# Local and downsampled attention ahead of two MLP layers: values loaded for two batches at once, and the turning of the probabilities moved one unit later

## The reference

```python
q_d = q.reshape(B, H, Sd, factor, D).mean(axis=3)        # factor 4: 144 positions; k_d, v_d alike
out_up = np.repeat(sm_attn(q_d, k_d, v_d), factor, axis=2)
mask = np.abs(pos[:, None] - pos[None, :]) < factor      # a band of 7 keys around each query
out_local = softmax(where(mask, scale * q @ k.T, -1e9)) @ v
x = rows_of(out_up + out_local)                          # 2304 x 512
xn = x / rms(x) * rms_g
x = (silu(xn @ w_gate) * (xn @ w_val)) @ w_out           # 512 -> 1536 -> 512
y = square(relu(x @ w_in)) @ w_out2                      # 512 -> 2048 -> 512
```

## Time and profile before

| | |
|---|---|
| median of 3 runs | 962.38 us (960.26 to 963.59) |
| the profiled execution | 963.09 us, of which the span in the profile is 961.3 us |
| mean granted TensorE clock | 0.978 of full speed |
| PE busy | 926.8 us, 96% of the span |
| attention units, up to the first product | about 143 us of the span |

### The profile page before, as it was taken

One profiled execution on the slowest core, in us unless ns is written; L12 is line 12 of the kernel. 1 busy time (PEld: TensorE's weight loads), 2 busy tenths in 40 slices (PEclk: granted clock), 3 DMA queues, 4 the chain that ended last, 5 costly groups with the idle time before them and its releaser, 6 DMA issues.

```text
span 961.3 us, 17765 instructions
## 1 busy us (share of the span) xinstructions
PE 926.8 (96%) x6056; PEld 837.6 (87%) x6056; DVE 648.3 (67%) x960; ACT 447.9 (47%) x1149; POOL 588.7 (61%) x627
## 2 busy tenths in 40 slices
PE   5879989999999999999999999999999999999998
PEld 5657768999999999999999998989898998989896
DVE  5859995678986668876455776667875456745353
ACT  3758785644455634455444464424342324333221
POOL 2458677778778867877766775555654445453520
PEclk9979878999999999999999999999999999999999
DMA  6566211321211111111111122121112101030101
GB/s 178 180 206 210 82 35 33 89 77 54 68 45 44 45 45 45 45 45 45 44 46 54 54 69 88 44 88 45 45 36 97 45 23 44 23 110 23 45 1 65
DMA packets 57961, 63.94 MB, mean 67 GB/s; under 512 B 5904, under 2 KB 50832, under 8 KB 57488
## 3 DMA queue, kind: packets, MB, share of 16 engines
q1 hardware_dynamic: 56288, 61.63, 20.8%
q10 hardware_dynamic: 1584, 1.18, 0.4%
HBM read 58.07 MB, written 4.72 MB: 65 GB/s over the span
## 4 chain that ended last, share of the span: by engine, by line
PE 77%; DVE 3%; issue 1%; ACT 1%; POOL 0%; DMA 0%; ACTq 0%; DVEq 0%
PE bank L1437 42%; PE bank L1492 20%; PE bank L1467 14%; DVE xs L1079 1%; ACT wst L698 0%; ACT xs L739 0%; DVE vt L1146 0%; DVE prod L1152 0%; PE bank L1447 0%; DVE wst L1086 0%; POOL wst L576 0%; DMA out_dram<-xT 0%; DVE gt L1146 0%; DVE wo L1191 0%; ACT xT L822 0%
## 5 line engine op out<-in xcount | busy, mean ns | idle before, releaser
L1437 PE MATMUL bank<-xs,wst 128*128 128x384 f32 x2520 | 505.1, 340 | 4.1 <-DVE vt L1146 2.4
L1437 PEld LDWEIGHTS bank<-xs,wst 128*128 128x128 f32 x2520 | 442.7, 189 | 28.6 <-issue 8.5
L576 POOL TENSOR_TENSOR wst<-wraw,wst 128x256 fp32r<-128x256 f32 x240 | 223.9, 952 | 143.0 <-ACT wst L698 141.7
L1492 PE MATMUL bank<-wo,gs 128*128 128x512 f32 x864 | 218.4, 393 | 1.4 <-ACT xT L822 0.8
L1467 PE MATMUL bank<-hb,wo 128*128 128x512 f32 x864 | 189.1, 336 | 1.3 <-DVE hb L1164 1.3
L1492 PEld LDWEIGHTS bank<-wo,gs 128*128 128x128 f32 x864 | 160.4, 188 | 29.8 <-DVE gs L1185 1.1
L1467 PEld LDWEIGHTS bank<-hb,wo 128*128 128x128 f32 x864 | 146.0, 188 | 9.9 <-issue 1.6
L1146 DVE TENSOR_TENSOR vt<-u,bank 128x384 f32<-128x384 f32 x120 | 66.2, 552 | 126.1 <-PE bank L1437 125.8
L698 ACT CAST wst<-wraw 128x256 fp32r<-128x256 f32 x360 | 123.1, 407 | 1.9 <-DMA wraw<-w_dram 1.2
L559 POOL TENSOR_TENSOR wraw<-wraw,stage 128x256 f32<-128x256 f32 x60 | 48.9, 815 | 96.5 <-DMA wraw<-w_dram 96.5
L785 ACT ACTIVATE sig<-gt 128x384 f32<-128x384 f32 x72 | 37.9, 526 | 124.8 <-DVE gt L1146 123.7
(11 more groups left out here) (110 smaller groups left out, 1054.5 us busy)
## 6 DMA issues: line engine op xcount, KB each, us to landing
wraw<-w_dram SPq DMA_DIRECT2D x180, 128.0 KB, 2.3
stage<-w_dram SPq DMA_DIRECT2D x60, 128.0 KB, 2.1
woraw<-w_dram SPq DMA_DIRECT2D x28, 256.0 KB, 3.0
vquad<-v_dram SPq DMA_DIRECT2D x16, 288.0 KB
out_dram<-xT SPq DMA_DIRECT2D x18, 256.0 KB, 2.9
vwin<-v_dram SPq DMA_DIRECT2D x56, 70.0 KB
kp<-k_dram SPq DMA_DIRECT2D x3, 1152.0 KB, 8.6
qs<-q_dram SPq DMA_DIRECT2D x3, 1152.0 KB, 11.0
```

What stands on the lines that cost most here:

```text
L576: nc.gpsimd.tensor_tensor(b[:, 1, :], w_source(w, p), b[:, 0, :].bitcast(fp32), ALU.subtract).then_inc(wlp_done, 1)
L1437: last = mm(XY[s % 2][:, 0:HC], wst[:, u % 2, p, pw, 128 * k:128 * k + 128], xs[:, p, px, k, :], start=(p not in CONTINUES and i == 0 and ...
L1492: last = mm(ACC[t][:, :], gs[:, v % 2, m, px, 128 * t:128 * t + 128], wo[:, 2 * j + m, pw, :], start=(j == 0 and n < 18 and i == 0), stop= ...
```

## The change

Four edits go together.

1. `LAG_T`, `LAG_V`, `LAG_O` go from 3, 4, 5 to 4, 5, 6. The rings of probabilities go from four to five. After the last pass one more turning, one more `values` and one more kept output are left over; they are written ahead of `product(0, 0)`.
2. The scores use four banks up to unit 32 (`FOUR_BANKS`), the fourth being `SS`, and then the same three as before. `bank_user(g)` gives the last unit that used a bank; `token_sums`, the first other user of `SS`, waits for unit 32's exponentials.
3. `load_v` asks for both batches of a window in one transfer, `load_vquad` for all rows of a batch: 9 and 2 transfers a group, not 18 and 4. The bytes and the 1 KB rows stay. The downsampled keys are written in another order, to match the values'.
4. DVE's low parts of the second weights move from passes 39 and 41 to 42 and 43; PE's first spread from 44 to 43, with ACT's copies left at 44 and 45; the first `normalise(0, k)` from 45 to 46; in the last group the downsampling one pass earlier. `outd` is placed elsewhere in SBUF.

```diff
-LAG_T, LAG_V, LAG_O = 3, 4, 5
-SRING = 4
-DRING = 4
+LAG_T, LAG_V, LAG_O = 4, 5, 6
+SRING = 5
+DRING = 5
+
+FOUR_BANKS = 33
...
-DVE_LOW_AT = ((24, 26), (39, 41))
+DVE_LOW_AT = ((24, 26), (42, 43))
...
-SPREAD_AT = (44, 45)
-NORM_AT = (45, 46, 47, 47)
+SPREAD_AT = (43, 45)
+KEEP_NORM_AT = (44, 45)
+NORM_AT = (46, 46, 47, 47)
...
-SUM_FOUR_AT = ((4, 6, 8, 9), (1, 3, 6, 9), (1, 3, 6, 9), (1, 3, 4, 9))
-SUM_V_AT = ((10, 11, 12), (10, 11, 12), (10, 11, 12), (5, 6, 7))
+SUM_FOUR_AT = ((4, 6, 8, 9), (1, 3, 6, 9), (1, 3, 6, 9), (0, 1, 3, 9))
+SUM_V_AT = ((10, 11, 12), (10, 11, 12), (10, 11, 12), (4, 5, 6))
...
-        TA, OA, SA = P[0:2], P[2:4], P[4:7]
+        TA, OA, SA = P[0:2], P[2:4], P[4:8]
...
         def score_bank(g):
-            return SA[(g + 2) % 3]
+            return SA[g % 4] if g < FOUR_BANKS else SA[(g + 2) % 3]
+
+
+        def bank_user(g):
+            return max((f for f in range(g) if score_bank(f) is score_bank(g)), default=None)
...
-                    for x in range(2):
-                        src = v_d[batch0(b) + x][t0:t1, D * head0(b):D * head0(b) + GC]
-                        sp.dma_start(vwin[b % 2][r0:r0 + t1 - t0, x, i, :], src).then_inc(done, 16)
+                    src = v_d[batch0(b):batch0(b) + 2, t0:t1, D * head0(b):D * head0(b) + GC]
+                    sp.dma_start(vwin[b % 2][r0:r0 + t1 - t0, :, i, :],
+                                 src.rearrange("x r n -> r x n")).then_inc(done, 16)
...
                 for x in range(2):
-                    for kt in range(2):
-                        v = v_d[batch0(b) + x][S // 2 * kt:S // 2 * kt + S // 2, D * head0(b):D * head0(b) + GC]
-                        sp.dma_start(vquad[:, kt, x, :, :],
-                                     v.rearrange("(p r) n -> p r n", r=FACTOR)).then_inc(vq_in, 16)
+                    v = v_d[batch0(b) + x][:, D * head0(b):D * head0(b) + GC]
+                    sp.dma_start(vquad[:, x], v.rearrange("(p r) n -> p r n", p=HK)).then_inc(vq_in, 16)
...
+            keep_output(G_ALL - 6)
+            take_turned(G_ALL - 4)
             first_copy(0)
...
                 pe.wait_ge(ss_add, 3)
+                pe.wait_ge(exp_done, FOUR_BANKS)
...
-                if g >= 3 and subtracted(g - 3):
-                    pe.wait_ge(sub_done, nth_subtracted(g - 3) + 1)
-                if g >= 3 and not subtracted(g - 3):
-                    pe.wait_ge(exp_done, g - 2)
+                old = bank_user(g)
+                if old is not None and subtracted(old):
+                    pe.wait_ge(sub_done, nth_subtracted(old) + 1)
+                if old is not None and not subtracted(old):
+                    pe.wait_ge(exp_done, old + 1)
...
+            transposes(G_ALL - 4)
+            values(G_ALL - 5)
             product(0, 0)
```

More of the change, by code:

```diff
@@ L154, in fused_kernel @@
         vwin[0] = sb("vwin0", [KW, 2, NL, GC], stack=att)
-        vquad = sb("vquad", [HK, 2, 2, FACTOR, GC], stack=att)
+        vquad = sb("vquad", [HK, 2, 2 * FACTOR, GC], stack=att)
         qs[1] = sb("qs1", [128, NH, S], stack=att)
@@ L759, in _ @@
                     squares(0, SQUARES_AT.index(g))
-                if g in SPREAD_AT:
-                    spread(SPREAD_AT.index(g))
+                if g in KEEP_NORM_AT:
+                    spread(KEEP_NORM_AT.index(g))
                 for p in range(NP):
@@ L974, in sum_four @@
                 if n % 2 == 0:
-                    src, dst = kp[b % 2][:, h, HALO:HALO + S], kd[:, h, :]
-                else:
-                    src, dst = qs[b % 2][:, h, :], qd[:, h, 0:SD]
-                nc.vector.reduce_sum(dst, src.rearrange("p a (s r) -> p a s r", r=FACTOR), AX).then_inc(ks_done, 1)
+                    src = kp[b % 2][:, h, HALO:HALO + S].rearrange("p a (s k r) -> p a k s r", k=2, r=FACTOR)
+                    dst = kd[:, h, :].rearrange("p a (k s) -> p a k s", k=2)
+                else:
+                    src = qs[b % 2][:, h, :].rearrange("p a (s r) -> p a s r", r=FACTOR)
+                    dst = qd[:, h, 0:SD]
+                nc.vector.reduce_sum(dst, src, AX).then_inc(ks_done, 1)
             def sum_values(b, n):
                 if n == 0:
-                    dve.wait_ge(vq_in, 64 * (b + 1))
+                    dve.wait_ge(vq_in, 32 * (b + 1))
                     ready(dve, pv_done, NU * b)
@@ L986, in sum_values @@
                     dve.wait_ge(vd_done, 3 * b + n)
-                first = vd[:, :, :, :] if n else vquad[:, :, :, 0, :]
-                nc.vector.tensor_tensor(vd[:, :, :, :], first, vquad[:, :, :, n + 1, :],
+                fours = vquad[:, :, :, :].rearrange("p x (k r) n -> p x k r n", k=2)
+                first = vd[:, :, :, :] if n else fours[:, :, :, 0, :]
+                nc.vector.tensor_tensor(vd[:, :, :, :], first, fours[:, :, :, n + 1, :],
                                         ALU.add).then_inc(vd_done, 1)
@@ L1384, in values @@
                     if b == 0 and i == 0:
-                        pe.wait_ge(v_part[0], 32 * V_PARTS[0])
+                        pe.wait_ge(v_part[0], 16 * V_PARTS[0])
                     if b == 0 and i == V_PARTS[0]:
-                        pe.wait_ge(v_part[1], 32 * (V_PARTS[1] - V_PARTS[0]))
+                        pe.wait_ge(v_part[1], 16 * (V_PARTS[1] - V_PARTS[0]))
                     if b == 0 and i == V_PARTS[1]:
-                        pe.wait_ge(v_in[b], 32 * (NL - V_PARTS[1]))
+                        pe.wait_ge(v_in[b], 16 * (NL - V_PARTS[1]))
                     if b > 0 and i == 0:
-                        pe.wait_ge(v_in[b], 32 * NL)
+                        pe.wait_ge(v_in[b], 16 * NL)
                     for x in range(2):
@@ L1405, in values @@
                             c = D * (2 * p + h)
-                            last = mm(output_bank(g)[halves[h], 0:SD], vd[:, kt, x, c:c + D],
+                            last = mm(output_bank(g)[halves[h], 0:SD], vd[:, x, kt, c:c + D],
                                       pdT[:, n % 2, kt, :, h, :], start=(kt == 0), stop=(kt == 1))
```

2 lines of the change are left out of this document (1 added, 1 removed).

## The result

The changed kernel takes **966.59 us** (median of 7 runs, 966.0 to 972.68), the kernel before 962.71 us in the same sessions (7 runs). The ratio is 1.0054 (95% interval 1.0028 to 1.008): slower by half a per cent, where 956.0 us were forecast. The profiled execution took 966.0 us, against 963.09 of the one before: 2.9 us more. The ratios leave out the executions of a slower state (a lower clock, over 10 us longer), the medians do not; only for e8 does that matter, and there both are given.

The account below looks back on a forecast made before the run. PE was taken to set the pace, with DVE nearly full and gains only in the first 150 us. 963.09 - 2.5 - 1.1 - 2.0 - 1.0 = 956.5, stated as 956.0 us after a 0.7 us median correction; 8-in-10 range 951.5 to 961.

Parts of the forecast that it names:

- What bounds the kernel: Whole kernel: PE sets the pace, DVE nearly full; gains lie in the first 150 us; longest PE stall 7.61 us for vwin.
- A: Value loads of group 1: joined transfers cut SP's issue time, so the awaited load lands 2.5 us earlier.
- B: Before the values of unit 13: scores of unit 18 move ahead of the stall, saving 1.1 us (0.9 to 1.3).
- E: Unit 34's bank, moved tables, leftover work before the first product, work behind the products: counted as 0 us.
- C: After 55 us: turning one unit later shortens four PE waits, 4.5 us together; 2.0 us taken, bounds 0 to 4.2.
- D: End of attention, up to about 151 us: PE enters without a 2.1 us wait; 1.0 us gained, bounds 0 to 3.3.
- the clock at the end comes back: Rival, 132 to 151 us: the clock is not at 0.50, giving about 952.5 us; chance 0.11.
- The load lands no earlier: Rival, value load of group 1: the single DMA engine is behind anyway, 2.5 us missing, 958.5 us; chance 0.18.
- Only B is left: Rival: waits reappear for a score bank or full DVE; only the extra unit ahead pays; about 961 us; chance 0.12.
- The slower case: Rival, after unit 13: PE stays at 1.2 GHz; with 20 us more of it about 966 us; chance 0.09.

Follow-up runs that it names:

- e8: Changed kernel with each 67-row edge window cut into 64 and 3 rows; 955.73 us over six executions, 953.8 us over the four its ratio of 0.9883 uses.
- e7: Kernel before with each 67-row window cut into transfers of 64 and 3 rows; 948.22 us, ratio 0.9824.
- e2: Changed kernel with the window and vquad loads of before, so the schedule change alone; 961.08 us, ratio 0.9987 to the kernel before.
- e9: Kernel before with joined windows and vquad in two transfers, edge windows cut into 64 and 3 rows; 957.17 us, ratio 0.9949.
- step 2: Four kernels, each the kernel before with one joined part: all windows, vquad, edge windows, middle windows; 963.36, 961.55, 962.22, 962.88 us.
- e1: Kernel before with the changed loads alone (joined windows, vquad in two transfers, keys' order to match); 965.2 us, ratio 1.0038.
- e3: Kernel before with only the windows of both batches joined, 9 transfers instead of 18, vquad in four; 963.36 us, ratio 0.9999.

## Why the prediction was wrong

**What bounds the kernel.** Right in most: the change acts in the first 150 us alone, DVE and PE are both full there, and the longest stall is the one for `vwin`. Wrong in the reason for it. The text read the two stages of the earlier trace rows as two limits one after the other: one engine alone until 37 us, then SP's issuing. But the lone engine doesn't end its work when the others start again: before, it was at work on the windows until 54.18 us, and the others had no piece of the windows left after 45.95. The last window to land goes through it as well. Share and GB/s are means over 16 engines; a load is done when its slowest engine is.

**A (-2.5 us).** The step that failed: "There SP's issuing is the limit", and from it "I take 2.5 us for the landing". The issue cost was sized well (0.41 us measured, 0.50 taken) and the last issue came 2.0 us earlier, but the landing came 3.1 us later, so this term alone is off by 5.6 us. The step rests on a row read wrongly: from 37.20 to 43.67 thirteen windows went out, 0.50 us each, not fourteen. The first of the fourteen was issued at 33.93 and took 3.22 us, that is, SP itself stood in the lone engine's stretch until 37.15. The sentence of A that held the truth, "The last window still has its 134 rows on one engine", was weighed for nothing. The rule of the Trainium skill ("DMA: Bandwidth & Descriptors", why a DMA increments its semaphore by 16) was cited for the number of engines and used for one stretch only. Its consequence, that 64 and 3 rows would run on 16 and 3 engines where 67 run on one, is what e7 tried: the trace agrees, with a share of 0.82 for 0.06. The Trainium skill's other rule ("DMA: Bandwidth & Descriptors", issuing engines are not separate DMA queues), that the time on the sequencer to start a DMA is usually small beside the DMA, agrees too: 0.57 us for the last window's issue stood beside 15.0 us until PE's release, and the issues saved brought nothing.

**B (-1.1 us).** The mechanism was right, the result was not a gain. The scores of unit 18 do stand ahead of the stall, and in e2 the stall is 2.1 us shorter, 1.6 of them by the work taken ahead. The stall ends when the load lands, so only work taken from behind it counts, and that work is given back before the first product: 6.8 us for 4.1 from the last downsampled scores to the product. The step that failed is in E, "The leftover turning and values ahead of `product(0, 0)` are the ones the loop did before". In number they are; but they now stand at the end, mostly at 1.2 GHz, where PE waits for them (1.45 and 1.68 us in the kernel after). Its rows from the last downsampled scores on:

```profile
138.62 0.95 PE L1368 MATMUL bank<-kd,qd 64*64 64x144 f32 x12
141.57 1.12 PE L1408 MATMUL bank<-probT,vwin 70*64 70x64 f32 x16 [1.45 <-ACT probT L675]
145.16 0.86 PE L1387 MATMUL bank<-ident,pd 128*72 128x128 f32 x3 [1.68 <-ACT probT L675]
147.00 2.29 PE L1450 MATMUL bank<-xs,wst 128*128 128x384 f32 x6
```

Before, one turning (at 140.35) and one unit's values (at 141.77) stood between the last downsampled scores at 138.71 and the product at 142.82.

**C (-2.0 us).** This term was mis-sized: the lower bound, nothing, was the true one. The waits after 55 us were 4.9 us in e2 for 5.1. They changed their names (`qd`, `probT`, a bank) and hardly their sum. The text had named the reason, a DVE that is full, and then taken the middle between the bounds.

**D (-1.0 us).** In the kernel after the clock is 0.74 from 132 to 151 us, for 0.50, which is the rival "the clock at the end comes back". It came behind the 4.1 us wait and a stretch at 1.2 GHz from about 124 to 131 us, where the kernel before had the full clock, so the term of 1.0 us can't be read from this trace.

**E (0).** Right for unit 34 (0.42 us) and the moved tables by themselves (e2: nothing lost that can be told). Missed was a collision: `SUM_V_AT` of the last group stands one pass earlier, with `vquad` 8.0 us later, and DVE takes nothing out of turn. The clause of A, "the 67-row blocks cost the same in all", held for the first window only: behind it SP stood for 10.21 us in one issue, where before it stood for 6.49 and 3.22 us in two. Behind the last window it failed: the first `vquad` transfer took 6.48 us, where before all four together took 5.61, and the lateness grew through the groups.

**The rivals.** "The load lands no earlier" had the right place and the right witness (26 GB/s), at 0.18; the argument against it, that this stretch ends before the 14 issues start, was the error of A again (the first of them stood in it). It stopped at zero, while the sign turned: the joined transfers made the load later. "Only B is left" describes e2. The slower case named a low clock after unit 13. There was a low stretch from 56 to 63 us, but the kernel before had one there too, from 49 to 59, and in sum the clock was equal, so that rival did not happen: 966 us is its number by luck, reached another way.

**What stays open.** Why the same rows take more engine time in joined transfers (3% over the whole queue in the kernel after, though e2 with single transfers has 1% too; 5 to 8% less rate in the first 30 us with both joined). Counted from the trace's completion records, the lone engine moved the 338 rows between the queries of group 1 and the last window in 17.3 us before and in 19.5 us after, 51 and 58 ns a row; 1.8 us of the 2.2 more fall on the rows up to the end of the middle windows. More neighbours at the same time would explain this, but not the 240 GB/s of e9 at a share of 0.98. The order in which a joined transfer walks through memory is a guess that no run here tests. That the waits at 141 and 145 us follow from the late group 3, and how the four single parts of step 2 add to the loads' 3.65 us, was not shown either.

## What to carry to other kernels

Before you speed up the issue of a load, ask which engine finishes it. Here a DMA share of 0.06 while a load was awaited belonged to transfers of 67 rows on one engine, and that engine stayed behind until the landing; cutting the odd rows off (64 + 3) paid, at the price of more issues. Merging transfers saved issue time only, and it cost rate. A longer distance between stages gave nothing here, where one engine was full: it moved a unit's work from one place to another, and the place at the end of the pipe must be counted too. When a schedule uses a buffer earlier, compare with when its load lands, not with when it is free.

## What was unexpected of the hardware

One engine set the landings of the first 57 us, and the cut gave 14 us for four more issues a group. PE at half clock for 30 us left no trace in the start of the first product, since its load came later anyway (e1 beside e3). SP, too, was held behind 67-row transfers: issues that cost 0.4 us elsewhere took 6.49 and 3.22 us one after the other in the kernel before, and 10.21 and 6.48 us behind the joined edge windows. And with all engines 0.96 to 0.98 busy the rate was 240 GB/s with both loads joined, and 252 to 259 with none.
